# A three-stage kernel (windowed attention, gated FFN, routed experts): three blocks of the commonest expert taken before the routing is complete, two sets of expert weights, and the first expert's lower parts shared by GpSimd and VectorE

## The reference, cut to what matters

```python
x = attention(q, k, v)                 # B=2, H=8, S=768, D=64: window of 16 keys + 24 block summaries, softmax
x = x.reshape(1536, 512)
h = maximum(maximum(x @ w1, x @ w2), x @ w3)        # 512 -> 768
x = h @ w_out                                       # 768 -> 512
# routed experts: N=1536 tokens, E=8 experts, F=1024
do_compute = x @ w_skip > 0
logits = x[do_compute] @ w_gate;  e_idx = argmax(logits);  gate = softmax(logits)[e_idx]
for e in range(8):
    y[e_idx == e] = gate * (maximum(x[e_idx == e] @ w1[e], 0) @ w2[e])
out = x;  out[do_compute] += y
```

## Time and profile before

| | us |
|---|---|
| median of 3 runs (lowest, highest) | 510.82 (510.63, 510.92) |
| the profiled execution | 509.29 |
| its span, first to last instruction | 507.4 |
| PE busy | 457.7 (90%) |
| DVE busy | 215.3 (42%) |
| ACT busy | 178.1 (35%) |
| POOL busy | 73.5 (14%) |

### The profile page before, as it was taken

One profiled execution on the slowest core, in us unless ns is written; L12 is line 12 of the kernel. 1 busy time (PEld: TensorE's weight loads), 2 busy tenths in 40 slices (PEclk: granted clock), 3 DMA queues, 4 the chain that ended last, 5 costly groups with the idle time before them and its releaser, 6 DMA issues.

```text
span 507.4 us, 9816 instructions
## 1 busy us (share of the span) xinstructions
PE 457.7 (90%) x3453; PEld 394.7 (78%) x3454; DVE 215.3 (42%) x509; ACT 178.1 (35%) x461; POOL 73.5 (14%) x81
## 2 busy tenths in 40 slices
PE   2799899999999999999999815898999999999984
PEld 1589789989998998999899614676777777777763
DVE  5867834543343444234022197346222222222471
ACT  2866534444333343333221116254222222222350
POOL 0311622230000001000000001010111111111111
PEclk9999999999999999999999956999999999999999
DMA  8994125311300301200200228637111111111000
GB/s 280 332 343 158 59 59 173 90 48 37 106 27 27 110 28 39 88 1 1 98 0 2 83 102 319 268 125 265 41 41 41 41 41 41 41 41 37 23 16 2
DMA packets 20671, 46.66 MB, mean 92 GB/s; under 512 B 3756, under 2 KB 7468, under 8 KB 20640
## 3 DMA queue, kind: packets, MB, share of 16 engines
q1 hardware_dynamic: 18240, 39.99, 23.3%
q0 software_dynamic: 2400, 6.24, 3.7%
HBM read 37.89 MB, written 9.96 MB: 94 GB/s over the span
## 4 chain that ended last, share of the span: by engine, by line
PE 80%; DVE 7%; issue 4%; DMA 3%; ACT 3%; DVEq 1%; SPq 1%; POOL 0%; ACTq 0%; POOLq 0%
PE bank L574 30%; PE pair L702 15%; PE bank L692 12%; PE bank L589 10%; PE bank L516 2%; PE bank L684 2%; PE pair L469 2%; PE bank L501 2%; PE bank L616 2%; DMA e_raw<-experts_dram 1%; DVE e_lo L1062 1%; PE pair L678 1%; DVE k_w L908 1%; DMA rows<-x_rows,index_next 1%; DMA k_all<-k_all_dram 1%
## 5 line engine op out<-in xcount | busy, mean ns | idle before, releaser
L574 PE MATMUL bank<-x_hi,w_hi 128*128 128x256 f32 x432 | 127.5, 295 | 2.5 <-DVE w_lo L952 1.9
L574 PE MATMUL bank<-x_hi,w_lo 128*128 128x256 f32 x432 | 122.2, 283 | 0.0
L574 PE MATMUL bank<-x_lo,w_hi 128*128 128x256 f32 x432 | 122.1, 283 | 0.0
L574 PEld LDWEIGHTS bank<-x_hi,w_hi 128*128 128x128 f32 x432 | 82.5, 191 | 6.8 <-DVE w_lo L952 2.5
L574 PEld LDWEIGHTS bank<-x_lo,w_hi 128*128 128x128 f32 x432 | 82.7, 191 | 0.0
L574 PEld LDWEIGHTS bank<-x_hi,w_lo 128*128 128x128 f32 x432 | 82.6, 191 | 0.0
L1208 DVE TENSOR_TENSOR u_lo<-bank,u_hi 128x512 fp32r<-128x512 f32 x28 | 19.3, 689 | 80.9 <-ACT u_hi L860 80.9
L702 PE MATMUL pair<-e_hi,u_hi 128*128 128x512 f32 x112 | 47.9, 428 | 4.6 <-DVE u_lo L1208 3.5
L1252 POOL TENSOR_TENSOR probs<-probs,rowinv 128x480 f32<-128x480 f32 x24 | 23.7, 986 | 188.4 <-DVE rowinv L937 188.4
L692 PE MATMUL bank<-e_hi,r_hi 128*128 128x512 f32 x112 | 46.6, 416 | 3.7 <-DVE e_lo L1062 2.1
L1296 POOL DMA_INDIRECT rows<-x_rows,index_next x16 | 17.3, 1080 | 218.4 <-DVE index_next L1211 144.5
(11 more groups left out here) (160 smaller groups left out, 734.6 us busy)
## 6 DMA issues: line engine op xcount, KB each, us to landing
e_raw<-experts_dram SPq DMA_DIRECT2D x24, 512.0 KB, 5.4
w_raw<-ffn_w_dram SPq DMA_DIRECT2D x7, 768.0 KB, 12.9
v_w<-v_dram SPq DMA_DIRECT2D x24, 192.0 KB, 3.0
k_all<-k_all_dram SPq DMA_DIRECT2D x8, 400.0 KB, 4.4
q_t<-q_dram SPq DMA_DIRECT2D x24, 128.0 KB, 3.7
x_rows<-y_rows SPq DMA_DIRECT2D x12, 256.0 KB, 2.7
out_dram<-y_rows SPq DMA_DIRECT2D x12, 256.0 KB, 2.6
v_nat<-v_nat_dram SPq DMA_DIRECT2D x3, 512.0 KB, 6.8
```

The lines of the kernel that those rows point to most:

```text
L574: mm = pe.matmul(ring_of(gr, n)[:, 0:GT], w_parts[a][:, f, (w * KD + k) * P:(w * KD + k + 1) * P], x_parts[c][:, gr % XS, k, :], start=i = ...
```

## The change

Routing begins in the sixth group, for the 1024 tokens of the first four groups (`EG = 4`, `ET = 8` columns of 128 tokens). The expert with the most of these tokens (`star`) is found on the chip. Its weights are loaded then, into SBUF that attention no longer needs, and `EB = 3` blocks of its tokens run as the first three, straight after the sixth group's products. The full routing leaves out the tokens that these blocks took (`taken`), puts the star expert first in the order, and its instructions stand between those of the three blocks. There are two sets of weight buffers: the next expert's chunks are loaded when the other set is free, and split during the last block of the expert before. POOL makes `e_lo` of chunks 0 to 3 of the star expert, DVE that of chunks 4 to 7. Six small constant loads move from the end of attention to its start.

```diff
+EB = 3
+BY_POOL = 4
+EG = 4
+ET = EG * GT // P
...
+            store_rows(EG)
             sp.wait_ge(x_lo_done, GQ)
+            sp.wait_ge(star_done, 1)
+            star = sp.value_load(star_list[0:1, 0:1], min_val=0, max_val=NE - 1)
+            for c in range(ECH):
+                sp.dma_start(part_of(e_raw[c], FIRST_SET),
...
+                    sp.wait_ge(e_lo_done, ECH * a)
+                    sp.wait_ge(expert_left, a)
                     for c in range(ECH):
...
             for n in range(UNITS - TPG):
                 unit(gr, n)
+                if n == 1:
+                    early_ranks()
+                if n == 9:
+                    early_found()
+                if n == 13:
+                    early_gates()
             down_unit(gr, 0)
             down_unit(gr, 1, last=True)
+            early_up(0, 0, range(KD))
...
```

```diff
+            early_choice()
+            for n in range(UNITS):
                 unit(GROUPS - 1, n)
+                if n == 2:
+                    early_star()
+                if n == 5:
+                    early_rows()
+                if n == 8:
+                    early_places()
+                if n == 10:
+                    early_gate_parts()
+                if n == 12:
+                    early_index()
+                if n == 16:
+                    first_expert_lo(4)
...
+            def now(b, gates, indices, column):
+                dve.wait_ge(result_left, AHEAD + b)
...
+                    now(EB + n, slot_gate, index, bass.ds(n, 1))
                     with dve.If(ends > 0):
+                        expert_lo(na, range(1))
+                    up_lo(EB + n, 0)
+                    with dve.If(ends > 0):
+                        expert_lo(na, range(1, 3))
+                    up_lo(EB + n, 1)
+                    rows_lo(EB + n + 1)
+                    keep(EB + n + 1)
+                    next_index(EB + n + 2)
+                    with dve.If(ends > 0):
+                        expert_lo(na, range(3, 5))
+                    add(EB + n)
+                    with dve.If(ends > 0):
+                        dve.sem_inc(expert_left, 1)
+                        expert_lo(na, range(5, ECH))
...
+            for c in range(BY_POOL):
+                pool.wait_ge(e_hi_done, c + 1)
+                pool.tensor_tensor(part_of(e_parts[1][c], FIRST_SET), part_of(e_raw[c], FIRST_SET),
+                                   part_of(e_parts[0][c], FIRST_SET).bitcast(F32), ALU.subtract
+                                   ).then_inc(e_lo_done_pool, 1)
+            stored(EG)
+            pool.wait_ge(route_ready, 1)
+            gather(0, EG * GT)
```

More of the change, by code:

```diff
@@ L203, in program @@
-        up = place("up", [P, EF], F32, "moe")
-        u_hi = place("u_hi", [P, KE, P], F32R, "moe")
-        u_lo = place("u_lo", [P, KE, P], F32R, "moe")
-        result = place("result", [P, DM], F32, "moe")
-        assert at["experts"] <= BASE + 2 * 4 * WPIECES * WCH
-        assert at["moe"] <= at["moe_end"]
-        assert at["rows"] <= at["top"] and at["ffn"] <= ROWS
-        assert max(at.values()) <= nc.sbuf_usable_end, at
+        v_all = [place(f"v_all{i}", [P, S], F32, "v_all") for i in range(2)]
@@ new lines, in program @@
+        rows_keep = place("rows_keep", [P, 2, DM], F32, "block")
+        u_hi = place("u_hi", [P, KE, P], F32R, "block")
+        u_lo = place("u_lo", [P, KE, P], F32R, "block")
+        result = place("result", [P, DM], F32, "block")
+        assert at["block"] <= at["top"]
+        h_a = place("h_a", [P, GT])
+        h_m = [place(f"h_m{i}", [P, GT]) for i in range(2)]
+        ident = place("ident", [P, P])
+        gate_w = place("gate_w", [P, KD, NE + 1])
+        logits = place("logits", [P, NT, NE + 1])
@@ new lines, in early_found, with early_gates @@
+            def early_found():
+                pe.wait_ge(a_places_done, 1)
+                for t in range(ET):
+                    mm = pe.matmul(a_ps_found[:], a_row_hot[:, t, :], a_places[:, t], start=t == 0, stop=t == ET - 1)
+                mm.then_inc(a_found_done, 1)
+            def early_gates():
+                pe.wait_ge(a_gates_at_done, 1)
+                for t in range(ET):
+                    mm = pe.matmul(a_ps_gates[:], a_row_hot[:, t, :], a_gates_at[:, t], start=t == 0, stop=t == ET - 1)
+                mm.then_inc(a_gates_found_done, 1)
@@ new lines, in early_up @@
+            def early_up(b, half, ks):
+                if half == 0:
+                    pe.wait_ge(r_hi_done, b + 1)
+                    pe.wait_ge(r_lo_done, b + 1)
+                for k in ks:
+                    pe.wait_ge(e_lo_done_pool, k + 1)
+                    for a, c in MM3:
+                        mm = pe.matmul(ps_up[half][:], (r_hi, r_lo)[a][:, k, :],
+                                       part_of(e_parts[c][k], FIRST_SET, half * 512, 512),
+                                       start=(k == 0 and a + c == 0), stop=(k == KD - 1 and a == 1))
+                if ks[-1] == KD - 1:
+                    mm.then_inc(up_done, 1)
@@ new lines, in up_product @@
+            def up_product(n, na, half, ks):
+                for k in ks:
+                    pe.wait_ge(e_lo_done, ECH * na + k + 1)
+                    for a, c in MM3:
+                        mm = pe.matmul(ps_up[half][:], (r_hi, r_lo)[a][:, k, :],
+                                       part_of(e_parts[c][k], set_of(na), half * 512, 512),
+                                       start=(k == 0 and a + c == 0), stop=(k == KD - 1 and a == 1))
+                if k == KD - 1:
+                    mm.then_inc(up_done, 1)
@@ new lines, in down_product @@
+            def down_product(n, na, fs):
+                for f in fs:
+                    pe.wait_ge(e_lo_done, ECH * na + KD + f // 2 + 1)
+                    for a, c in MM3:
+                        mm = pe.matmul(ps_down[:], (u_hi, u_lo)[a][:, f, :],
+                                       part_of(e_parts[c][KD + f // 2], set_of(na), f % 2 * DM, DM),
+                                       start=(f == 0 and a + c == 0), stop=(f == KE - 1 and a == 1))
+                if f == KE - 1:
+                    mm.then_inc(down_done, 1)
@@ L649, in _ @@
             mm.then_inc(turned, 1)
+            early_up(0, 1, range(2))
+            turn_up(0, 0)
             pe.wait_ge(turned_copied, 2 * TPG * GROUPS - 1)
```

807 lines of the change are left out of this document (530 added, 277 removed).

## The result

The changed kernel takes **506.93 us** (median of 7 runs, 505.48 to 508.45), the kernel before in the same rounds 510.63 (7 runs, 509.19 to 513.97). The ratio is 0.992, with an interval of 0.989 to 0.995: a gain of 3.7 us, where I had forecast 10.5, and outside my range of 493.5 to 505.5. The profiled execution takes 506.31, its span is 504.5, against 509.3 and 507.4 before.

What follows compares the result with a forecast made beforehand. Bound by matmuls, with one hole of 27.6 us. From 287.6, added work and waits, 177.8 of block products, expert changes, end and clock gave a 496.9 span; with 1.9 and 1.5 more, 500.3 us, range 493.5 to 505.5.

Steps and rivals of the forecast that it cites:

- the clock: TensorE's clock may fall at the waits of 5.1 and 4.5 us; half of 1.4 counted twice, +1.4 us.
- the wait in block 1: Second early block: u_lo, behind scatter landing and tables, comes later than TensorE wants it, +4.5 us (3.4 to 5.5).
- the end: From 500.12 to the span's end at 507.4 in the kernel before: 7.3 us, kept in the sum.
- the part before 249 us: Constant loads and VectorE setup lie under attention, where VectorE is idle over half the time: nothing, at most 2 us.
- rival (b): More waits, for a_places, ring maxima or routing in block 1: adds 3 to 8, 503 to 508 us; chance 0.13.
- Rival (a): GpSimd is no hindrance to VectorE, or one chunk's worth only: 494.4 to 497.9 us; chance 0.27.
- (d): Early blocks not full, or star's remainder needing 9 blocks: a 15th block, 12.7 us, 513; chance within a shared 0.06.
- The sixth group: Before block 0: small matmuls and transposes +1.8, row split +0.65, wait for a_places behind GpSimd's chunks 5.1 us.
- Steady blocks: Loop blocks stay near 12.70 us; scatter wait ahead of u_lo just covered, 0.1 in 8 blocks, +0.8 us.
- Rival (c): Scatter landing in 3.9 instead of 2.8 puts u_lo 0.9 late in 11 blocks: 511.3 us; chance within a shared 0.06.
- Changes of expert: Two in the loop, with a split ahead of u_lo and a late scatter: 3.2 us each, 6.4 against 7.0 before.
- Block 0 and 2: First early block: transposes, logits and ranks, +1.95 us; third: gates and 0.2 of scatter wait, +1.0 us.

Runs made afterwards that it cites:

- The branch: Against the changed kernel, TensorE branches once per loop block on the weight set, so matmuls have fixed addresses: 504.08 us, ratio 0.987.
- the version with all waits late: Changed kernel with VectorE making all eight chunks, every scatter wait behind its block's splits, 16 loop turns, branch on the set: 483.03 us, ratio 0.945.

## Why the prediction was wrong, point by point

The failing steps were terms of the sum, not the plan. Two were mis-sized: the clock (1.4 us, measured 5.1) and the wait in block 1 (4.5, measured 6.1). Three were put at nothing or copied: the register addresses of the second set (3.1 against 0.8 that I had given to something else), the end (1.3), and the part before 249 us (1.1). Together they are 10 us; the sum is only 7.6 short because other terms were too dear by some 2.4, which is luck.

The time fell into the band of rival (b), 503 to 508, but for none of its reasons: only two chunks came ahead of `a_places`, no maximum was waited for, and the list of experts was written 16.2 us after block 0 began, where I had 16.4. Rival (a) is out by the 4.67 us at unit 9, (d) by the 14 blocks.

- **The sixth group: right in mechanism and size.** "Ready at 271.4, a wait of 5.1": it was 271.59 and 4.67. The gap at unit 9, the order of the two engines and the price of a chunk (2.4; the one that was asked for during `a_row_hot` took 2.71) were as forecast. The run with VectorE alone shows that this half of the change costs 6.1 us.
- **The clock: the term that was mis-sized most.** I wrote "I count half of that twice: +1.4". It fell in full at three waits, not two: 24 matmuls took 4.96 in place of 2.97 (2.0), six products and four transposes 3.74 in place of 2.09 (1.7), and at the second change of expert 2.61 and 0.87 in place of 1.63 and 0.44 (1.4). Together 5.1. The first block before had told a price, 1.4; nothing told me to halve it. It is no constant either: behind the same wait at unit 9 other executions lost 1.4 to 2.2 us, and block 1 lost 1.7 to 2.9 behind waits of 3.5 to 6.1. Where the wait of 4.7 or of 6.1 is taken out, the clock stays at 1.00.
- **Block 1: "3.9, as the second expert's load starts beside it".** I named the collision and priced it by the worst landing before. It was 5.08, and in other arrangements 7.0 to 8.5. That is 1.2 of the 2.9 us; 1.7 is the clock above. A slip hides in the sum too: 22.2 + 0.4 + 1.67 + 0.6 + 0.69 is 25.6, not 25.3, so my own terms gave 4.8; the rest of the block was 0.4 shorter than I had it.
- **Steady blocks: "nothing" for the second set.** I priced the double set by buffers and loads, not by how TensorE finds it. Register addresses with their arithmetic cost 0.28 a block in 11 blocks, 3.1 us, of which my 0.8 for another cause covered a part. This is the bound that I had set myself (longer than 12.8), and it was crossed. The branch shows it.
- **Rival (c), the scatter sets the block:** right as a mechanism, 0.15 us a block behind the arithmetic, but not active in the change. Its price of 0.9 was too high for steady blocks, because landing takes 2.8 there.
- **Changes of expert: the first one right by luck.** It took 28.5 against 28.7, but 0.6 of that are the register addresses of its two blocks, counted above; the stall itself is 2.5, where I had 3.2. **The second one is 2.0 short**: a scatter lies beside the third expert's load and landed in 4.0 us in place of 2.8. That made the waits 0.65 longer than at the first change, and the clock added 1.4. I had said for block 1 that a load makes a landing late, and did not ask where the third load would fall.
- **The end: "7.3", copied.** Three more empty turns add 1.25, about 0.4 each. Here the loop is the last thing that runs, and its turns that do nothing cost time.
- **Before 249 us: "nothing, at most 2":** 1.07, within the bound, 0.8 to 0.9 of it the setup on VectorE. "VectorE is idle more than half the time" was no cover; which due time of the attention step was missed there, no run shows, and the other 0.2 is open.
- **Block 0 and 2** were 0.4 and 0.45 too dear.

The sign was right and the hole at 290 to 316 is filled. None of the 7.6 us that came on top of my sum is work of the matmuls, and nearly all of it, with the two waits that I had forecast, can be had back: the version with all waits late is 24 us faster than the change.

Of "GPSIMD Engine Reference", section "Key points", in the Trainium skill I had cited the contention for VectorE's instructions with two SBUF inputs. It also names instructions in a two-port mode. The trace agrees with more than I used: `a_lsum_e` and the cast `a_gate_b` have one tensor input each and took 2.22 and 2.09 us beside GpSimd, the reciprocal 0.20; whether the first two ran in that mode, no row shows. The Trainium skill's "SBUF — State Buffer", section "SBUF: two separate sides", says that the one who begins first keeps the pair of ports for its whole instruction; the rows agree, as each held step ends within 0.3 us of the end of a chunk: `h_lo` at 267.97 and the chunk at 267.68, `a_lsum_e` at 272.29 and the chunk (in equal thirds of 7.11) at 272.25.

The Trainium skill's "DMA: Bandwidth & Descriptors", section "Queues, rings and completion order", says that each DMA engine takes turns between its queues, packet by packet. The landings of 5.08, 8.14 and 8.47 us beside loads, against 2.8 alone, show that taking turns does not keep a scatter short here. The section goes on to the order of completion, which I had not taken into account; what holds the landing back, no run here shows.

## What to carry to other kernels

Ask of every wait what is queued behind it on its engine, and put a wait for a store's landing behind all work that others need; placed so, a late landing cost no time here, whereas moving the load only moved the collision. Look at the gathers too: one that fell beside the load cost 1.7 us. Where VectorE and GpSimd get in each other's way, as here, price each small step by the other engine's whole instruction, and give the work to the engine that has room for it (VectorE, in the run with all eight chunks) before the one that is merely idle. When a buffer becomes one of two, look at the issuing engine's instruction stream too, and count the empty turns of a loop whose work was moved elsewhere.

## What the runs showed of the hardware that I had not expected

- A scatter of 128 rows landed in 2.8 us alone and later beside eight loads of 512 KB (some 420 GB/s), by where it lay among them: 4.8 to 5.3 when it began 0.3 us ahead of their first, 8.47 when its own instruction was slow there, 7.0 to 8.14 when it began 3.5 us behind it, 3.5 to 5.5 some 10 us behind it.
- A gather of 128 rows beside the same loads took 7.69 us, where the median in the change is 3.4.
- GpSimd's scatter instruction itself took 1.94 us in place of 1.01 when VectorE ran `row_hot` (1.75 us) beside it.
- A wait of 4.7 us on TensorE cost 2.0 us more for the clock. It was still at 1.00 some 2 us into the wait, at 0.50 from 270 to 276, and 0.80 from 276 to 277, after TensorE had been busy again since 271.65.
- Register arithmetic ahead of matmuls of 0.23 us each is mostly hidden; 0.21 us show in the first 18 products of a block and 0.08 at the first down product.
